# Three early tiles of the most chosen expert, not two, in a fused attention, channel-mix and expert kernel

## The reference

```python
logits = x2 @ w_gate                      # 8 per token
fresh_e = argmax(logits[b, s])
e = fresh_e if s == 0 or local_gate[b, s] < 0.5 else prev_e
p = softmax(logits[b, s])
h = maximum(x2[b, s] @ w1[e], 0)          # 512 -> 1024
out[b, s] = p[e] * (h @ w2[e])            # 1024 -> 512
```

## Time and profile before

| | before |
|---|---|
| median of 3 runs | 621.07 us (619.95 to 621.63) |
| the profiled execution | 621.54 us, of which its span is 619.5 |
| TensorE matmuls busy | 608.2 us (98%) |
| DVE, ACT, POOL busy | 410.9, 321.4, 178.9 us |
| mean granted TensorE clock | 0.999 of full speed |

### The profile page before, as it was taken

One profiled execution on the slowest core, in us unless ns is written; L12 is line 12 of the kernel. 1 busy time (PEld: TensorE's weight loads), 2 busy tenths in 40 slices (PEclk: granted clock), 3 DMA queues, 4 the chain that ended last, 5 costly groups with the idle time before them and its releaser, 6 DMA issues.

```text
span 619.5 us, 14715 instructions
## 1 busy us (share of the span) xinstructions
PE 608.2 (98%) x4483; PEld 505.0 (82%) x4484; DVE 410.9 (66%) x1164; ACT 321.4 (52%) x698; POOL 178.9 (29%) x257
## 2 busy tenths in 40 slices
PE   8999999999999999999999999999999999999996
PEld 6878888888888888889979878788788888888885
DVE  4767779845888797786979958957736235463541
ACT  5767779777516614632544844637526125362531
POOL 4545545600000000000000331585732521544141
PEclk9999999999999999999999999999999999999999
DMA  8987886002210010000004661786933522764000
GB/s 308 377 278 245 266 284 219 18 2 86 63 74 0 1 51 18 0 34 35 0 23 166 239 235 51 287 306 215 339 124 118 201 65 84 251 208 144 17 17 15
DMA packets 32935, 84.66 MB, mean 137 GB/s; under 512 B 4602, under 2 KB 7418, under 8 KB 32896
## 3 DMA queue, kind: packets, MB, share of 16 engines
q1 hardware_dynamic: 26816, 70.03, 32.5%
q0 software_dynamic: 3200, 8.92, 4.3%
q10 hardware_dynamic: 2880, 5.24, 2.6%
HBM read 76.04 MB, written 9.70 MB: 138 GB/s over the span
## 4 chain that ended last, share of the span: by engine, by line
PE 93%; DVE 4%; issue 1%; ACT 0%; POOL 0%; DVEq 0%; POOLq 0%; ACTq 0%
PE banks L889 23%; PE banks L891 23%; PE banks L890 23%; PE banks L760 4%; PE banks L827 3%; PE banks L1079 3%; PE banks L836 2%; DVE we_lo L1531 2%; PE banks L790 2%; PE banks L774 2%; PE banks L804 1%; PE banks L800 1%; PE banks L998 1%; PE banks L851 1%; PE banks L792 1%
## 5 line engine op out<-in xcount | busy, mean ns | idle before, releaser
L1498 DVE CUSTOM_DVE_ANT_0 product<-x,xT 128x512 f32<-128x512 f32 x120 | 77.9, 688 | 1.4 <-DMA xT<-in_w 1.3
L1800 ACT ACTIVATE prob<-neg,negmax 128x160 f32<-128x160 f32 (+1 forms) x136 | 59.2, 436 | 29.9 <-DVE negmax L1209 20.2
L1778 DVE TENSOR_SCALAR hid<-banks 128x512 f32<-128x512 f32 x34 | 23.5, 691 | 72.7 <-PE banks L891 71.6
L1910 ACT ACTIVATE k_sum<-banks 128x512 f32<-128x512 f32 (+2 forms) x40 | 21.4, 534 | 88.2 <-PE banks L891 84.7
L889 PE MATMUL banks<-we_hi,hid_hi 128*128 (+1 forms) x160 | 66.6, 416 | 0.2 <-DVE hid_lo L1611 0.2
L889 PE MATMUL banks<-we_hi,xg_hi 128*128 (+1 forms) x160 | 64.7, 404 | 0.9 <-DVE we_lo L1531 0.9
L686 POOL MEMSET xg<- 128x1024 f32 x1 | 1.0, 953 | 218.6 <-ACT k_raw L1903 218.6
L891 PE MATMUL banks<-we_hi,hid_lo 128*128 (+1 forms) x160 | 62.6, 392 | 0.0
L891 PE MATMUL banks<-we_hi,xg_lo 128*128 (+1 forms) x160 | 62.6, 391 | 0.0
L890 PE MATMUL banks<-we_lo,hid_hi 128*128 (+1 forms) x160 | 62.5, 391 | 0.0
L890 PE MATMUL banks<-we_lo,xg_hi 128*128 (+1 forms) x160 | 62.4, 390 | 0.0
(11 more groups left out here) (295 smaller groups left out, 1471.3 us busy)
## 6 DMA issues: line engine op xcount, KB each, us to landing
xT<-in_w_e SPq DMA_DIRECT2D x36, 512.0 KB, 4.6
raw_end<-in_w_e SPq DMA_DIRECT2D x36, 512.0 KB, 5.0
qk<-in_qk_t SPq DMA_DIRECT2D x32, 448.0 KB, 6.3
vw<-in_v_t SPq DMA_DIRECT2D x32, 256.0 KB, 5.6
w_raw<-in_w_mix ACTq DMA_DIRECT2D x20, 256.0 KB, 3.9
x_rows<-x SPq DMA_DIRECT2D x17, 256.0 KB, 2.0
xT<-in_w SPq DMA_DIRECT2D x8, 256.0 KB, 3.4
vz<-in_v_z SPq DMA_DIRECT2D x8, 128.0 KB, 3.7
```

Source lines behind the costliest of these rows:

```text
L1498: dve.tensor_tensor_reduce(product[:, k % 2, :], x2[:, t, :], w9(e), 1.0, 0.0, ALU.mult, ALU.add, dot[:, t % 2, e:e + 1]).then_inc(dotted, 1)
L1778: dve.tensor_scalar(hid[:, D * h:D * (h + 1)], ps_h[:, h, :], 0.0, None, ALU.max).then_inc(hid_ready, 1)
L1800: act.activation(prob[:, t % 2, c], neg[:, c], ACT.Exp, scale=-1.0, bias=negmax[:, t % 2, k:k + 1], accum_out=rsum[:, t % 2, k:k + 1]).the ...
```

## The change

EARLY becomes 3. Three tiles of the first expert are given slots in the mix, and tile 2 is the third of them; tile 3, in the loop, becomes the first tile of expert 0. DVE sorts the early slots in three tiles (third, past_first, in_third). POOL gathers tile 2 when the rows of tile 0 have been turned, before its weight parts of the first expert, for which it no longer waits for DVE's. Weight parts 6 and 7 of r = 1 go from DVE to POOL, and all parts of r = 2 into the loop. keep_clock between the tiles is left out, and turn_rows(2) goes into tile 1. The steps of the choice are placed later in the list of TensorE, and DVE's and ACT's lists are reordered around them; the table is now made behind rest_of_rows(3).

```diff
-EARLY = 2
+EARLY = 3
@@ gpsimd
-            for b in range(EARLY):
+            for b in range(2):
                 gather(b, b, NA * P)
-            pool.wait_ge(we_lo_ready, VPARTS + VPARTS)
+            pool.wait_ge(xg_turned, 1)
+            gather(2, 0, NA * P)
             last_parts(0, slice(0, 1))
...
-            for b in range(EARLY):
-                pool.wait_ge(xg_turned, b + 1)
-                gather(EARLY + b, b, TOK)
+            pool.wait_ge(xg_turned, 2)
+            gather(3, 1, TOK)
             pool.wait_ge(xg_turned, 3)
             gather(4, 0, TOK)
-            for b in range(EARLY):
+            for b in range(2):
                 scatter(b, b)
-            pool.wait_ge(we_last_lo_ready, 3 * LPARTS)
-            last_parts(2, slice(0, 1))
+            last_parts(1, slice(1, 2))
@@ tensor
-            hidden(0, first, 1, range(2, 3))
-            turn_keeps(final)
-            hidden(0, first, 1, range(3, DC)).then_inc(hid_summed, 1)
+            hidden(0, first, 1, range(2, DC)).then_inc(hid_summed, 1)
             turn_rows(1, 1, 0)
             pe.wait_ge(we_lo_ready, VPARTS + VPARTS)
             outputs(0, 0, first, range(0, 1))
+            turn_keeps(final)
+            turn_hidden(0, 1)
+            outputs(0, 0, first, range(1, 3))
             turn_last_runs(final)
-            turn_hidden(0, 1)
+            outputs(0, 0, first, range(3, 5))
             turn_carries(final)
-            outputs(0, 0, first, range(1, 3))
+            outputs(0, 0, first, range(5, 7))
             turn_chosen(final)
-            outputs(0, 0, first, range(3, 4))
-            count_picks(final)
-            outputs(0, 0, first, range(4, FC)).then_inc(y_summed, 1)
+            outputs(0, 0, first, range(7, FC)).then_inc(y_summed, 1)
...
-            hidden(1, first, 0, range(DC)).then_inc(hid_summed, 1)
+            hidden(1, first, 0, range(0, 1))
+            count_picks(final)
+            hidden(1, first, 0, range(1, DC)).then_inc(hid_summed, 1)
...
-            find_slots()
+            turn_rows(2, 0, 1)
             pe.wait_ge(y_copied, 1)
             outputs(1, 0, first, range(0, 1))
             turn_hidden(1, 1)
-            outputs(1, 0, first, range(1, FC)).then_inc(y_summed, 1)
-            turn_rows(2, 0, 1)
-            keep_clock(IDLE_TURNS // 4)
-            other = slice(1, 2)
-            pe.wait_ge(we_lo_ready, VPARTS + PARTS // 2 + VPARTS)
+            outputs(1, 0, first, range(1, 6))
+            find_slots()
+            outputs(1, 0, first, range(6, FC)).then_inc(y_summed, 1)
...
+            hidden(2, first, 1, range(DC // 2, DC)).then_inc(hid_summed, 1)
             sum_gates()
+            pe.wait_ge(y_copied, 2)
+            outputs(2, 0, first, range(1))
+            turn_hidden(2, 1)
+            outputs(2, 0, first, range(1, 2))
             turn_rows(3, 1, 1)
+            outputs(2, 0, first, range(2, FC)).then_inc(y_summed, 1)
@@ vector
+                parted = done(dve.tensor_scalar(third[:], place_early[:], float(2 * P), None, ALU.is_ge))
...
-                        to = min(at + (3 if tiles == GT else 1 if f < GT and last_group(g) else 2), left)
+                        to = min(at + (3 if tiles == GT else (0, 1, 1, 1, 2, 2, 2, 2)[f] if last_group(g) else 2), left)
...
-            for j in range(PARTS // 2, VPARTS):
+            rest_of_part(0, slice(0, 1), PARTS // 2)
+            last_x2(1)
+            for j in range(PARTS // 2 + 1, VPARTS):
                 rest_of_part(0, slice(0, 1), j)
-            last_x2(1)
...
+            rest_of_hidden(0, 0)
             dve.tensor_tensor(ldiff[:], logit[:, :, 0:E], by_token(lmax[:], E), ALU.subtract).then_inc(diff_ready, 1)
-            rest_of_hidden(0, 0)
             runs(final)
+            rest_of_hidden(0, 1)
             carries(final)
-            rest_of_hidden(0, 1)
+            rest_of_rows(1)
             choices(final)
-            rest_of_rows(1)
+            rest_of_part(1, slice(1, 2), 0)
...
+            rest_of_hidden(1, 0)
...
+            rest_of_hidden(1, 1)
...
+            rest_of_rows(2)
+            rest_of_part(1, slice(1, 2), 1)
             dve.wait_ge(route_pe, 12)
             slots(slot_of, LATER, slot_token[:, EARLY:MT])
...
+            rest_of_hidden(2, 0)
+            rest_of_part(1, slice(1, 2), 2)
             dve.wait_ge(gates_summed, 1)
...
-            for j in range(VPARTS, PARTS):
-                rest_of_part(1, slice(1, 2), j)
-            rest_of_hidden(2, 0)
+            rest_of_part(1, slice(1, 2), 3)
+            rest_of_hidden(2, 1)
+            rest_of_rows(3)
...
-            rest_of_rows(3)
-            rest_of_hidden(2, 1)
-            for j in range(VPARTS):
-                rest_of_part(2, slice(0, 1), j)
+            for j in range(PARTS // 2, VPARTS):
+                rest_of_part(1, slice(1, 2), j)
...
-            with dve.Fori(EARLY + 1, MT) as i:
+            with dve.Fori(EARLY, MT) as i:
@@ scalar
             relu_hidden(2, 0)
             round_hidden(2, 0)
+            relu_hidden(2, 1)
+            round_hidden(2, 1)
...
             act.wait_ge(gates_ready, 1)
-            weigh_y(0)
-            relu_hidden(2, 1)
+            for b in range(2):
+                weigh_y(b)
             round_rows(3)
```

More of the change, by code:

```diff
@@ L288, in program @@
         second = sb("second", [P, NA], to=second_half)
+        third = sb("third", [P, NA], to=second_half)
+        past_first = sb("past_first", [P, NA], to=second_half)
+        in_third = sb("in_third", [P, NA], to=second_half)
         slot_early = sb("slot_early", [P, NA], to=second_half)
@@ L1133, in _ @@
             turn_hidden(1, 1)
-            outputs(1, 0, first, range(1, FC)).then_inc(y_summed, 1)
-            turn_rows(2, 0, 1)
-            keep_clock(IDLE_TURNS // 4)
-            other = slice(1, 2)
-            pe.wait_ge(we_lo_ready, VPARTS + PARTS // 2 + VPARTS)
+            outputs(1, 0, first, range(1, 6))
+            find_slots()
+            outputs(1, 0, first, range(6, FC)).then_inc(y_summed, 1)
             pe.wait_ge(xg_lo_ready, 4)
             pe.wait_ge(hid_ready, 5)
-            hidden(2, other, 0, range(DC)).then_inc(hid_summed, 1)
+            hidden(2, first, 0, range(DC)).then_inc(hid_summed, 1)
+            pe.wait_ge(hid_ready, 6)
+            hidden(2, first, 1, range(DC // 2))
+            turn_hidden(2, 0)
+            hidden(2, first, 1, range(DC // 2, DC)).then_inc(hid_summed, 1)
             sum_gates()
[L1145 to L1148, removed]
+            pe.wait_ge(y_copied, 2)
+            outputs(2, 0, first, range(1))
+            turn_hidden(2, 1)
+            outputs(2, 0, first, range(1, 2))
             turn_rows(3, 1, 1)
[L1150 to L1154, removed]
+            outputs(2, 0, first, range(2, FC)).then_inc(y_summed, 1)
             pe.wait_ge(tables_ready, 1)
@@ L1428, in early_onehots @@
                                                         ALU.mult, ALU.add))
-                in_second = done(dve.tensor_tensor(by_tile_early[:, :, 0, 1], taken[:, 0:NA], second[:], ALU.mult))
-                after(slotted)
+                done(dve.tensor_tensor(past_first[:], taken[:, 0:NA], second[:], ALU.mult))
+                after(slotted, parted)
+                done(dve.tensor_tensor(in_third[:], taken[:, 0:NA], third[:], ALU.mult))
+                after(done(dve.scalar_tensor_tensor(slot_early[:], third[:], -float(P), slot_early[:], ALU.mult, ALU.add)))
                 dve.wait_ge(mix_hi_ready, 2 * DC * GROUPS)
@@ L1436, in early_onehots @@
                                            by_token(slot_early[:, c0:c1], P), ALU.is_equal))
-                after(in_second)
-                after(done(dve.tensor_tensor(by_tile_early[:, :, 0, 0], taken[:, 0:NA], by_tile_early[:, :, 0, 1],
-                                             ALU.subtract)))
+                done(dve.tensor_tensor(by_tile_early[:, :, 0, 0], taken[:, 0:NA], past_first[:], ALU.subtract))
+                done(dve.tensor_tensor(by_tile_early[:, :, 0, 1], past_first[:], in_third[:], ALU.subtract))
+                after(done(dve.tensor_copy(by_tile_early[:, :, 0, 2], in_third[:])))
                 dve.tensor_tensor(by_tile_early[:, :, 1, :], by_tile_early[:, :, 0, :], by_token(iota_tile[:, 0:NA], EARLY),
@@ L1619, in _ @@
             fresh_choice(final)
+            rest_of_hidden(0, 0)
             dve.tensor_tensor(ldiff[:], logit[:, :, 0:E], by_token(lmax[:], E), ALU.subtract).then_inc(diff_ready, 1)
-            rest_of_hidden(0, 0)
             runs(final)
+            rest_of_hidden(0, 1)
             carries(final)
-            rest_of_hidden(0, 1)
+            rest_of_rows(1)
             choices(final)
-            rest_of_rows(1)
+            dve.wait_ge(x2_turned, 2)
+            for t in range(2):
+                dve.wait_ge(x2_stored[t], 16 * GROUPS)
+            rest_of_part(1, slice(1, 2), 0)
             dve.wait_ge(route_pe, 10)
@@ L1680, in _ @@
```

(17 more changed lines are left out.)

13 lines of the change are left out of this document (1 added, 12 removed).

## The result

The changed kernel takes 631.5 us (629.6 to 632.64, 6 runs) beside 621.24 (619.95 to 622.23, 6 runs) for the kernel before on the same chip: a ratio of 1.0163, 95% interval [1.0142, 1.0184]. That is 10.3 us slower; the forecast was 620.7 us. The profiled execution took 632.64 us, with a span of 630.8.

A forecast was written before the change was run, and what follows sets the result against it. TensorE, holding 93% of the chain of waits, was taken as the bound. An earlier loop start (-0.8 us) and a longer single tile (+0.4) made -0.4, from a median of 621.07 to 620.7 us; range 617.6 to 622.7.

The forecast's parts named there:

- The seam: Between the second and third hand-written tiles: TensorE's stop, with its idle transposes, goes, saving 2.7 us.
- The number of tiles, the moved slots: Total stays 20 tiles, 17 in the loop; finding slots within the second tile is in time by 0.8 us.
- P0: Moment the third tile's first matmul starts, forecast at 387.3.
- port contention: DVE's weight parts beside POOL's lose 0.35 us each, costing nothing to +0.3; rival with late slots: 621.5, chance 0.11.
- the small steps: Shifts on the way to P0 from x2, keep transposes, choice steps and row transposes, summed to -0.5 us.
- first stop of +0.35: New TensorE stop where x2 comes late, at 354.6 instead of 354.23, behind DVE's extra slot operations.
- Parts 6 and 7 by POOL: Expert 0's weight parts made about P0 + 18, needed at P0 + 25, so they cost nothing.
- The table's chain: At the loop's start: table ready at P0 + 13.4, first matmul 2.7 us later with TensorE empty.
- The clock as a rival: Clock falls in the stop at the loop's start: +2.6 us, 623.2 to 623.7, chance 0.08.
- The single tile: Loop tile behind expert 4's only one takes 12.77 us instead of 12.36, as behind expert 1's: +0.4 us.
- what the forecast called -0.4: Net change of the whole kernel: -0.8 us at the loop's start, +0.4 for the single tile.
- The rivals on the slower side: Clock falling at the loop's start (623.2 to 623.7, chance 0.08); late slots or port contention (621.5, chance 0.11).

The follow-up runs named there:

- e7: e5 with DVE's two weight parts put back ahead of the second x2 tile: 620.15 us, ratio 0.9987.
- e3: Changed kernel, POOL again waiting for DVE's parts of the first expert and DVE making expert 0's parts 6 and 7: 623.39 us, ratio 1.0045.
- e5: e3 with the tile table made earlier, ahead of the third tile's first hidden part: 621.05 us, ratio 0.9997.
- e2: Changed kernel, with DVE instead of POOL making weight parts 6 and 7 of expert 0, behind the table: 624.84 us, ratio 1.0063.
- e10: Changed kernel with the table's conversion written as an addition of zero in the same place: 631.7 us, ratio 1.0164.
- e12: Kernel before, without the nine idle transposes between its tiles: 622.61 us, ratio 1.0018.
- e6: Changed kernel with only the tile table made earlier, ahead of the third tile's first hidden part: 623.98 us, ratio 1.0049.
- e9: Changed kernel where the table's last arithmetic operation writes the integers itself, so the conversion is gone: 623.92 us, ratio 1.0047.
- e4: Kernel before, without the wait that puts POOL's first two weight parts behind DVE's: 625.75 us, ratio 1.0073.
- e8: e3 with 18 idle transposes ahead of TensorE's wait for the table: 621.64 us, ratio 1.001.

## Why the prediction was wrong, point by point

- **The seam (-2.7): right.** After, the third tile's first matmul starts at 391.73, 0.23 us behind its neighbour, with no stop.
- **The number of tiles, the moved slots: right.** find_slots (389.71) waits for nothing.
- **P0 (387.3): wrong by 4.4 us, 391.73.** The step that failed is the sentence on port contention: "DVE's may lose 0.35 each ... nothing, up to +0.3". It took its price from the spread in the earlier trace rows, which comes from the loop. There, too, POOL's four operations lie back to back, but DVE's two lengthened parts (432.83 and 436.03, 1.28 and 1.56 us) began 0.2 and 0.5 us ahead of the end of one of them and waited for that end alone; the 2.27 to 2.37 us in POOL's rows are its own waits for a part of DVE. So the spread showed how late in a hold these parts happened to begin, and not how long a hold can be. In the mix's last tiles the price was 4.7 us for the pair (7.03 less 2.35). 3.2 us of it reached TensorE, as a stop and as half clock: the first tile's first hidden transposes start 14.03 us behind the x2 transposes, 10.82 before. The row of before at 360.37, POOL's four halves in 5.0 us, could not show it either: the wait that the change removes kept DVE's parts out of it. Another place of that trace did show a hold through a whole run, the other way round, and I had not read it (DVE, POOL):
```profile
401.09 4.61 DVE L1531 TENSOR_TENSOR we_lo<-xT,we_hi 128x1024 fp32r<-128x1024 f32 x4
405.63 2.34 DVE L1531 TENSOR_TENSOR we_lo<-raw_end,we_hi 128x1024 fp32r<-128x1024 f32 x2
...
401.74 7.12 POOL L680 DMA_INDIRECT out_rows<-y,rows_out  x1 [1.68 <-ACT y L2003]
```
The scatter before it took 1.03 us; this one stood until DVE's six parts were over. With the first loss out of the way (e7), P0 stands at 33.72 behind the first x2 transposes, against 33.6 for the same place before; the sum of the small steps (-0.5 behind a first stop of +0.35, so -0.85) was too good by 1 us, 0.35 of it the order that e7 puts back.
- **"Parts 6 and 7 by POOL ... nothing": wrong, 5.34 us.** I asked when the parts are needed, and not what DVE does while POOL makes them; and I put them at P0 + 18, where they began at P0 + 13.5 (405.24 less 391.73), beside the table's last operation at P0 + 12.95.
- **The table's chain: right.** Table ready at P0 + 13.4, loop 2.7 later. Measured without the hold (e3): P0 + 13.14 (402.46 less 389.32), and 2.50. In the changed kernel the table would have been ready at 404.85, P0 + 13.12, and the loop follows its true end at 410.19 by 2.50 again. That the table was late there at all cost 2.4 us (the loop starts at P0 + 15.64 in e3 and P0 + 13.25 in e7), where the forecast had 2.7, and an early place for it was free (e5).
- **The clock as a rival (0.08): mechanism right, bound wrong.** It was priced from a stop of 3.6 us, "it decides from a stop that reaches toward that". Here it came behind 1.90 us. Of nine stops of 1.90 to 2.21 us in these profiles, five were followed by half clock (the changed kernel, e2's second, e3, e10, e12) and four were not (e2's first, e6, both of e9). A stop of 2.67 us (e4) was followed by it too. The price was right in size: 3 us for six at the lower pace, 1.6 measured for 3.4 (e3 and e8).
- **The single tile (+0.4): there, but of twice the size.** From the first hidden transposes of the tile behind expert 4's single one to those of the next are 13.19 us in the changed kernel and 12.35 at the same place before; behind expert 1's they are 13.13, and 12.76 before. That the rest of e8 is only 0.41 us longer than before's is partly luck: other tiles came out shorter.

Sum: 3.2 (first loss) + 5.34 (the held table) + about 1.9 (half clock in the loop: 218.11 less e9's 216.25) = 10.4 of 10.66. What is left, +0.2, is what the forecast called -0.4. The rivals on the slower side held one of the mechanisms each, the contention at about a tenth of its size (0.7 to 1 us against 3.2 and 5.34), with 0.19 for the two together.

Of a VectorE operation with both inputs in SBUF, or a copy, cast or tensor_scalar in its two-port form, beside a GpSimd one, the Trainium skill says in SBUF — State Buffer (Who interferes with whom) that the one issued first gets the shared pair and "the other fully blocks". The prediction cited this and rejected it by the earlier trace rows; the runs bear it out for the weight parts, the conversion, the addition and the choice's two operations, and for the relu that reads PSUM, which it lets pass. Whether the conversion and the addition ran in that two-port form no trace shows. My price by it was 0.7 us because I let it hold for one instruction of POOL. That is how long it held in e4 and for the choice's two operations in e3; at the two places of the loss four in a row kept hold (5.89 us for one part, 5.51 for the conversion), and no run here shows why.

## What to carry to other kernels

When work moves to POOL, list what DVE issues during it, operation by operation, and ask of each whether all its inputs lie in SBUF; work out the time with a hold of one instruction of POOL and with one of its whole back-to-back run, since both came here, and don't take the price from the spread of durations elsewhere, which depends on when the operations happened to begin. Look for the reverse too: a row of either engine that is far longer than its neighbours of the same form. A wait that looks like mere order ("POOL after DVE's parts") may be what keeps the two apart. A tiny operation on which another engine's control flow hangs, such as a table that a loop reads, belongs where its engine stands idle anyway, and a stop of about 2 us ahead of matmuls brought the half clock in five of nine cases here.

## What the runs showed that I had not expected

- An operation on 24 numbers took 5.51 us (0.17 free of the run), in both forms that were tried, and 0.2 us of start time separate it from the one ahead of it that ran free: 0.77 us ahead of POOL's first recorded operation, and 0.57.
- The hold goes both ways: a COPY of one number per partition on POOL took 3.62 us beside four weight parts of DVE (e3), 0.20 otherwise:
```profile
403.43 3.62 POOL L679 COPY rows_out<-slot_token 128x1 uint32<-128x1 uint32 x1 [0.59 <-DMA out_rows<-y,rows_out]
```
- A stop of 1.90 us can be followed by 1.2 GHz, and need not be. The changed kernel, e2, e6, e9 and e10 are the same on TensorE up to their first stop, which is 1.90 to 1.92 us long and ends 6.9 us behind the first x2 transposes in each; the clock fell in the changed kernel and e10 and stayed at 1.00 in the other three. So the length of the stop alone does not decide it.
- From the table's end to the loop's first matmul TensorE needs 2.50 us when nothing hides it (after, e3), 2.49 in e2, and 2.68 in e9, where it was still busy when the table came.
